# Block means of the values, made and sent in the pair's own first step

## The chip, the cores and the metric

The kernel runs on one core of one Trainium2 chip. The metric is the device time of one execution in microseconds, the median of several runs. The engines are named as the profile names them: PE (TensorE), DVE (VectorE), ACT (ScalarE), POOL (GpSimd) and SP (SyncE). Each works through its own list of instructions in order. An instruction that must wait for another engine holds everything behind it in its list.

## The reference

Three layers follow each other: an attention over 2 x 8 heads of 768 positions and 64 columns, a mixture of experts over the 1536 tokens (8 experts, two per token), and a dense layer with a leaky ReLU. The change touches only the attention:

```python
block, window = (32, 16)
k_sum = k.reshape(B, H, nb, block, D).max(axis=3)
v_sum = v.reshape(B, H, nb, block, D).mean(axis=3)
mask_l = np.abs(pos[:, None] - pos[None, :]) < window
scores_s = scale * np.einsum('bhsd,bhnd->bhsn', q, k_sum) + np.log(block)
...
a = softmax(np.concatenate([scores_l_m, scores_s], axis=-1))
return np.matmul(a, np.concatenate([v, v_sum], axis=2))
```

Each position attends to its near neighbours and to 24 block summaries. The summary of the values is their mean over 32 rows. These means are what the change is about.

## The kernel before

Two heads are a pair. There are 8 pairs (n = 0 to 7), and each has three steps (groups of four units of 64 positions), so 24 steps c = 3n, 3n+1, 3n+2. One step passes through five stages that are spread over neighbouring steps in the lists of the engines:

- `score(c)` on PE, line 1229: products of queries and keys.
- `softmax_max(c)` on DVE, lines 876 and 880: scale, mask and row maximum.
- `softmax_exp(c)` on ACT, line 666: four exponentials.
- `turn_probs(c)` on PE, line 1238, and `probs_out(c)` on ACT, line 674: transpose and copy out.
- `weigh(c)` on PE, line 1259: products with the values, then `normalise(c)` on DVE, lines 911 to 925.

Beside this, each pair has its queries and keys turned (`turn_q`, line 1186, `turn_k`, line 1195), the turned keys copied by ACT (`k_part`, lines 679 and 680) and the block maxima of the keys copied by ACT (`k_means`, line 685). From pair 2 on, `gate_turn` (line 1283) turns the results of an older pair for the router. It writes into the bank from which `k_part` reads, so it waits until the key copy of the next pair is done (`k_ready`).

The values of a pair lie in `v_win`, one of three buffers, with 120 rows: 64 own ones, 32 of the neighbours, and 24 block means. The means of pair n >= 1 travel like this. PE multiplies the values by a matrix of 1/32 (`block_means`, line 1207, 8 instructions at the head of a `score`). DVE copies the sums out (line 885, behind the row maximum). ACT issues three small transfers of 8 rows each (`means_out`, line 696), which bring them to the right rows. POOL spreads them over the units of `v_win` (line 582, in `finish_windows`). `weigh(3n)` waits for that (`windows_ready`). The table `MEANS_AT` says in which step the means of each pair are made.

Three queues matter around it. POOL's list is: for each pair, two copies of neighbour rows (lines 577, 579), the spread, then pieces of the first expert's weights, which are split into two parts (lines 528, 530). Two pieces stand behind the spreads of pairs 5 and 7, one behind those of pairs 2, 3, 4 and 6. SP loads the values of pair n+2 when `weigh(3n-1)` is done, then queries, keys and weights. At the end of the attention SP waits until the means of pair 7 have landed, and loads the noise and six more pieces of weights behind that.

Of the kernel before, what the change touches and what calls it, by code (L numbers as in the profile page):

```python
# [29 lines left out]
PAIRS = B * H // 2  # L30
# [3 lines left out]
GROUPS = UNITS // GU  # L34
# [6 lines left out]
BANK = 512  # L41
MEANS_COL = 256
MEAN_LOADS = 3
MEANS_AT = {2: 1} | {GROUPS * n - 2: n for n in range(2, PAIRS)}
THIRD = UNITS // 4
MASKED = -1e9
EPS = 1e-9
# [27 lines left out]
def build(nc, q, k, v, w_gate, w_noise, noise, w1, w2, w_in, w_out, out):  # L75
    ctx = ExitStack()
    with ctx:
# [580 lines left out]
        def _(act):  # L658
# [3 lines left out]
            def softmax_exp(c):  # L662
                b = c % 2
                act.wait_ge(max_ready, c + 1)
                for u in range(GU):
                    last = nc.scalar.activation(probs[:, b, u, :], scores[:, b, u, :], ACT.Exp, bias=negmax[:, b, u:u + 1])  # L666
                last.then_inc(probs_ready, 1)

            def probs_out(c):
                b = c % 2  # L670
                act.wait_ge(probs_turned, c + 1)
                if c >= 2:
                    act.wait_ge(weighed, c - 1)
                nc.scalar.copy(probsT[:, b, :], t_bank[b][0:KC, :]).then_inc(probsT_ready, 1)

            def k_part(n):

                act.wait_ge(k_turned, n + 1)
                nc.scalar.copy(kT[:, n % 2, :, 0:AFTER], k_own_after)
                nc.scalar.copy(kT[:, n % 2, :, AFTER:WK], k_ahead).then_inc(k_ready, 1)  # L680

            def k_means(n):

                act.wait_ge(k_max_done, n + 1)
                nc.scalar.copy(kT[:, n % 2, :, WK:KC], k_max[:].unsqueeze(1).to_broadcast([P, UNITS, NB])).then_inc(k_max_ready, 1)

            def means_out(n):

                act.wait_ge(means_copied, n)
                if n > VBUF:  # L690
                    act.wait_ge(windows_ready, n - VBUF)
                row, put = mean_parts[:].ap[0][0], mean_rows[:].ap[0][0]
                for u in range(THIRD):
                    of = bass.AP(mean_parts, (n % 2 * THIRD + u) * 2 * D, [[16 * row, 8], [1, 2 * D]])
                    to = bass.AP(mean_rows, (WK + 8 * u) * put + n % VBUF * 2 * D, [[put, 8], [1, 2 * D]])
                    act.dma_start(to, of).then_inc(means_loaded[n % VBUF], 16)

            def gate_xT(m, first=0, end=TPB):

                cols = slice(first * P, end * P)  # L700
                nc.scalar.copy(xT_gate[:, cols], turned[:, cols]).then_inc(gate_xT_ready, 1)
# [6 lines left out]
            for n in range(PAIRS):  # L708
                c = GROUPS * n
                if c >= 1:  # L710
                    probs_out(c - 1)
                softmax_exp(c)
                if c - 1 in MEANS_AT:
                    means_out(MEANS_AT[c - 1])
                if n == 0:
                    act.wait_ge(first_means_done, 1)
                    nc.scalar.copy(v_win[WK:KC, 0, :, :, 0:D], first_mean_bank.rearrange("x (h d) -> x h d", h=2).unsqueeze(2).to_broadcast([NB, 2, UNITS, D])).then_inc(first_means_ready, 1)
                elif n + 1 < PAIRS:
                    k_part(n + 1)

                probs_out(c)
                softmax_exp(c + 1)
                if c + 1 - 1 in MEANS_AT:
                    means_out(MEANS_AT[c + 1 - 1])
                if n == 0:
                    k_part(1)
                if n >= 2:
                    act.wait_ge(gate_turned, n - 1)
                    act.wait_ge(gate_multiplied, n - 2)
                    gate_xT(n - 2)  # L730

                probs_out(c + 1)
                if n + 1 < PAIRS:
                    k_means(n + 1)
                softmax_exp(c + 2)
                if c + 2 - 1 in MEANS_AT:
                    means_out(MEANS_AT[c + 2 - 1])
            act.wait_ge(gate_turned, PAIRS - 1)
            act.wait_ge(gate_multiplied, PAIRS - 2)
            gate_xT(PAIRS - 2)  # L740
# [858 lines left out]
```

## Time and profile before

| What | Value |
|---|---|
| Median of 3 runs | 788.01 us (785.98 to 790.22) |
| Profiled execution, its own time | 780.19 us |
| Span in the trace | 778.6 us |
| PE busy | 757.3 us, 97% of the span |
| DVE, ACT, POOL busy | 262.1, 230.2 and 368.8 us |
| Attention stage, from the trace | about the first 103 us |

The page of the profile gives averages over three stages that have little in common. The attention fills the first eighth of the span. In it the work of a step passes from PE to DVE to ACT and back. In the rest of the span PE works almost without a gap. An instruction in the rows below is read as start, length, engine, line, operation, what it writes and reads, and how many were merged. The brackets say how long its engine stood idle before it, and what ended that. `ACTq` rows are transfers that ACT's sequencer issues, and their length is the time that the issue takes, not the transfer.

### The profile page before, as it was taken

What the parts mean: (1) busy time and instruction counts of PE and PEld (TensorE: products, weight loads), DVE (VectorE), ACT (ScalarE), POOL (GpSimd) and SP (SyncE); (2) the same over time, 40 slices, a digit from 0 to 9 for tenths busy, and PEclk for the clock granted to TensorE, in tenths of its full rate; (3) what the DMA queues carried; (4) which work ended last, traced back from release to release, by engine and by line L of the source; (5) the groups of instructions that cost most, each with busy time, mean ns of one, the idle gap of its engine ahead of it and who ended that gap; (6) DMA issues with size and microseconds to landing.
All of it is one profiled execution on the core that took longest, in us unless ns stands there. A gap on an engine that the chain in (4) does not pass through costs nothing.

```text
span 778.6 us, 13087 instructions
## 1 busy us (share of the span) xinstructions
PE 757.3 (97%) x4497; PEld 619.8 (80%) x4498; DVE 262.1 (34%) x457; ACT 230.2 (30%) x384; POOL 368.8 (47%) x313
## 2 busy tenths in 40 slices
PE   8888899999999999999999999999999999999998
PEld 6666667788888888888888888888888888888886
DVE  2787772122221212222122221165443334332223
ACT  3677772212212122221212212144222222221221
POOL 5277836579787687879388852810110001000000
PEclk8899999999999999999999999999999999999999
DMA  9699766983544526262544612261110101010001
GB/s 183 124 243 218 219 225 211 338 289 121 183 154 99 212 93 207 90 215 95 175 162 139 200 65 61 88 231 53 29 54 28 54 4 51 0 54 0 0 1 54
DMA packets 77041, 97.74 MB, mean 126 GB/s; under 512 B 45768, under 2 KB 49008, under 8 KB 76976
## 3 DMA queue, kind: packets, MB, share of 16 engines
q1 hardware_dynamic: 58832, 45.52, 21.0%
q0 software_dynamic: 12464, 43.79, 17.6%
q10 hardware_dynamic: 5712, 7.99, 2.8%
q8 instruction: 21, 0.34, 0.2%
q14 instruction: 12, 0.10, 0.0%
HBM read 75.43 MB, written 23.59 MB: 127 GB/s over the span
## 4 chain that ended last, share of the span: by engine, by line
PE 90%; DVE 3%; DMA 2%; ACT 2%; SPq 1%; issue 1%; ACTq 0%; DVEq 0%
PE p L1426 43%; PE p L1531 6%; PE p L1533 6%; PE p L1532 6%; PE p L1546 5%; PE p L1548 5%; PE p L1547 5%; PE p L1418 3%; DMA v_win<-in_v 2%; PE p L1413 2%; PE p L1381 1%; ACT scores L666 1%; DVE scores L876 1%; PE p L1238 1%; PE p L1229 1%
## 5 line engine op out<-in xcount | busy, mean ns | idle before, releaser
L565 POOL TENSOR_TENSOR w_lo<-stage,w_hi 128x1024 fp32r<-128x1024 f32 x56 | 134.1, 2395 | 4.7
L1426 PE MATMUL p<-w_hi,hT_hi 128*128 x240 | 96.5, 402 | 0.0
L1426 PE MATMUL p<-w_hi,xT_hi 128*128 x240 | 96.1, 400 | 0.3 <-DVE xT_lo L1071 0.3
L1426 PE MATMUL p<-w_lo,hT_hi 128*128 x240 | 93.9, 391 | 0.0
L652 POOL DMA_INDIRECT y_pick<-y_by_tile,slots x20 | 19.2, 959 | 157.6 <-PE p L1518 132.4
L1426 PE MATMUL p<-w_lo,xT_hi 128*128 x240 | 93.6, 390 | 0.0
L1426 PE MATMUL p<-w_hi,hT_lo 128*128 x240 | 93.6, 390 | 0.0
L1426 PE MATMUL p<-w_hi,xT_lo 128*128 x240 | 93.5, 390 | 0.0
L1531 PE MATMUL p<-f_xT_hi,w_hi 128*128 (+2 forms) x200 | 77.2, 386 | 0.8 <-DVE f_xT_lo L1115 0.8
L796 ACT CAST hT_hi<-p 128x1024 fp32r<-128x1024 f32 x30 | 30.5, 1016 | 155.7 <-PE p L1418 155.7
L1533 PE MATMUL p<-f_xT_hi,w_lo 128*128 (+2 forms) x200 | 76.2, 381 | 0.0
L1532 PE MATMUL p<-f_xT_lo,w_hi 128*128 (+2 forms) x200 | 76.2, 381 | 0.0
L1546 PE MATMUL p<-w_hi,f_hT_hi 128*128 128x512 f32 x192 | 74.8, 390 | 0.1
L1548 PE MATMUL p<-w_hi,f_hT_lo 128*128 128x512 f32 x192 | 74.7, 389 | 0.0
L1547 PE MATMUL p<-w_lo,f_hT_hi 128*128 128x512 f32 x192 | 74.7, 389 | 0.0
L1123 DVE SCALAR_TENSOR_TENSOR f_h<-p,f_h 128x512 f32<-128x512 f32 x48 | 33.2, 691 | 119.9 <-ACT f_h L826 119.9
L1071 DVE TENSOR_TENSOR xT_lo<-p,xT_hi 128x512 fp32r<-128x512 f32 x31 | 21.4, 691 | 147.5 <-ACT xT_hi L793 147.5
L791 ACT ACTIVATE h_row<-p 128x1024 f32<-128x1024 f32 x30 | 30.8, 1027 | 135.6 <-PE p L1426 129.5
L826 ACT COPY f_h<-p 128x512 f32<-128x512 f32 x48 | 28.2, 588 | 143.3 <-PE p L1533 143.3
L563 POOL TENSOR_SCALAR w_hi<-stage 128x1024 fp32r<-128x1024 f32 x56 | 59.2, 1057 | 15.1 <-DMA stage<-in_moe_w 12.4
L1077 DVE COPY y_row<-p 128x512 f32<-128x512 f32 x31 | 21.5, 694 | 116.7 <-PE p L1426 116.7
L1426 PEld LDWEIGHTS p<-w_lo,hT_hi 128*128 128x128 f32 x240 | 45.0, 188 | 10.0
(231 smaller groups left out, 1288.1 us busy)
## 6 DMA issues: line engine op xcount, KB each, us to landing
stage<-in_moe_w POOLq DMA_DIRECT2D x48, 512.0 KB, 4.2
w_land<-in_moe_w SPq DMA_DIRECT2D x16, 512.0 KB, 5.6
y_by_tile<-y_row ACTq DMA_DIRECT2D x29, 256.0 KB, 2.0
x_by_tile<-x_ring SPq DMA_DIRECT2D x28, 256.0 KB, 4.9
x_row<-x_by_tile SPq DMA_DIRECT2D x28, 256.0 KB, 3.2
v_win<-in_v SPq DMA_DIRECT2D x8, 384.0 KB, 5.7
x_tokens<-x_out SPq DMA_DIRECT2D x12, 256.0 KB, 5.6
out<-f_y SPq DMA_DIRECT2D x9, 256.0 KB, 2.0
```

Of the source, the lines that this page charges most:

```text
L563: pool.tensor_scalar(w_hi[:, par, cols], stage[:, c % STAGES, :], 1.0, 1.0, ALU.mult, ALU.mult).then_inc(hi_split, 1)
L565: pool.tensor_tensor(w_lo[:, par, cols], stage[:, c % STAGES, :], w_hi[:, par, cols].bitcast(F32), ALU.subtract).then_inc(lo_split, 1)
L791: nc.scalar.activation(h_row[:], h_bank[:], ACT.Relu).then_inc(h_ready, 1)
L796: nc.scalar.copy(hT_hi[:].rearrange("p c m -> p (c m)"), hT_bank[:]).then_inc(hT_hi_ready, 1)
L1123: nc.vector.scalar_tensor_tensor(out=h, in0=f_h_bank[c % 2], scalar=0.01, in1=h, op0=ALU.mult, op1=ALU.max).then_inc(f_leaky_done, 1)
L1426: last = nc.tensor.matmul(bank, a, w, start=(c == 0 and i == 0), stop=(c == left_hi.shape[1] - 1 and i == 2))
L1531: nc.tensor.matmul(to, hi, f_xT_hi[:, cols], start=(k == 0), stop=False)
L1532: nc.tensor.matmul(to, hi, f_xT_lo[:, cols], start=False, stop=False)
L1533: last = nc.tensor.matmul(to, lo, f_xT_hi[:, cols], start=False, stop=(k == KD - 1))
L1546: nc.tensor.matmul(f_y_bank[m], f_hT_hi[:, c % 2, rows], hi, start=(c == 0), stop=False)
L1547: nc.tensor.matmul(f_y_bank[m], f_hT_hi[:, c % 2, rows], lo, start=False, stop=False)
L1548: last = nc.tensor.matmul(f_y_bank[m], f_hT_lo[:, c % 2, rows], hi, start=False, stop=(c == FC - 1))
```

## The change

The table of steps is new, and ACT now looks up the current step instead of the one before. Nothing else is changed.

```diff
-MEANS_AT = {2: 1} | {GROUPS * n - 2: n for n in range(2, PAIRS)}
+MEANS_AT = {GROUPS * n: n for n in range(1, PAIRS)}
...
                 softmax_exp(c)
-                if c - 1 in MEANS_AT:
-                    means_out(MEANS_AT[c - 1])
+                if c in MEANS_AT:
+                    means_out(MEANS_AT[c])
...
                 probs_out(c)
                 softmax_exp(c + 1)
-                if c + 1 - 1 in MEANS_AT:
-                    means_out(MEANS_AT[c + 1 - 1])
...
                 softmax_exp(c + 2)
-                if c + 2 - 1 in MEANS_AT:
-                    means_out(MEANS_AT[c + 2 - 1])
```

Before, the means of pair 1 were made in step 2 and those of pair n >= 2 in step 3n-2, and their transfers were issued one step later, behind the exponentials of step 3 and of step 3n-1. Now both happen in step 3n. The lists of POOL and SP are the same as before.

PE's list before, around the means of pair 5 (line 1207) in step 13; line 1229 is a score and line 1259 a weighing, line 1283 the gate turn:

```order
L1207 MATMUL p<-v_win,half_sums 32x192 x8
L1229 MATMUL p<-kT,qT 64x120 x8
L1238 MATMUL p<-ident,scores 120x128 x4
L1283 MATMUL p<-ident,x_out 128x128 x6
L1259 MATMUL p<-v_win,probsT 64x65 x8
L1229 MATMUL p<-kT,qT 64x120 x8
L1238 MATMUL p<-ident,scores 120x128 x4
L1186 MATMUL p<-ident,qk_nat 128x128 x6
L1259 MATMUL p<-v_win,probsT 64x65 x8
L1229 MATMUL p<-kT,qT 64x120 x8
```

PE's list in the changed kernel, the same place (its lines are numbered 4 lower, so 1203 are the means, 1225 a score, 1279 the gate turn):

```order
L1225 MATMUL p<-kT,qT 64x120 x8
L1234 MATMUL p<-ident,scores 120x128 x4
L1279 MATMUL p<-ident,x_out 128x128 x6
L1255 MATMUL p<-v_win,probsT 64x65 x8
L1225 MATMUL p<-kT,qT 64x120 x8
L1234 MATMUL p<-ident,scores 120x128 x4
L1182 MATMUL p<-ident,qk_nat 128x128 x6
L1255 MATMUL p<-v_win,probsT 64x65 x8
L1203 MATMUL p<-v_win,half_sums 32x192 x8
L1225 MATMUL p<-kT,qT 64x120 x8
```

The eight products of the means of pair 5 stood before `score(13)` and now stand before `score(15)`, the first of their own pair.

ACT's list before, from the third step of pair 4 into pair 5 (line 666 are the exponentials, 696 the three issues, 679 and 680 the key copy, 674 the probabilities):

```order
L685 COPY kT<-k_max 128x12x24
L666 ACTIVATE scores<-scores,negmax 128x120 x4
L696 DMA mean_rows<-mean_parts 8x128 x3
L674 COPY probsT<-p 120x512
L666 ACTIVATE scores<-scores,negmax 128x120 x4
L679 COPY kT<-p 128x12x80
L680 COPY kT<-p 128x12x16
L674 COPY probsT<-p 120x512
L666 ACTIVATE scores<-scores,negmax 128x120 x4
L701 COPY xT_gate<-p 128x768
```

ACT's list in the changed kernel, the same place:

```order
L685 COPY kT<-k_max 128x12x24
L666 ACTIVATE scores<-scores,negmax 128x120 x4
L674 COPY probsT<-p 120x512
L666 ACTIVATE scores<-scores,negmax 128x120 x4
L696 DMA mean_rows<-mean_parts 8x128 x3
L679 COPY kT<-p 128x12x80
L680 COPY kT<-p 128x12x16
L674 COPY probsT<-p 120x512
L666 ACTIVATE scores<-scores,negmax 128x120 x4
L701 COPY xT_gate<-p 128x768
```

The three issues stood between the exponentials of step 14 and the copy-out of that step's probabilities. Now they stand between the exponentials of step 15 and the key copy of pair 6.

## Rows read from the trace of the kernel before

**Rows 1.** Timeline of PE, pair 5: start us, busy us, instruction, count.

```profile
66.39 0.64 PE L1229 MATMUL p<-kT,qT 64*64 64x120 f32 x16
...
69.93 0.86 PE L1207 MATMUL p<-v_win,half_sums 64*32 64x192 f32 x16
70.72 0.64 PE L1229 MATMUL p<-kT,qT 64*64 64x120 f32 x16
71.29 0.65 PE L1238 MATMUL p<-ident,scores 128*120 128x128 f32 x4
71.78 0.82 PE L1283 MATMUL p<-ident,x_out 128*128 128x128 f32 x6
72.53 0.69 PE L1259 MATMUL p<-v_win,probsT 120*64 120x65 f32 x16
...
74.89 0.85 PE L1186 MATMUL p<-ident,qk_other 128*128 128x128 f32 x6
75.67 0.69 PE L1259 MATMUL p<-v_win,probsT 120*64 120x65 f32 x16
76.28 0.64 PE L1229 MATMUL p<-kT,qT 64*64 64x120 f32 x16
```

**Rows 2.** Timeline of PE: the two means that waited for values.

```profile
60.05 0.86 PE L1207 MATMUL p<-v_win,half_sums 64*32 64x192 f32 x16 [1.69 <-DMA v_win<-in_v]
...
80.50 0.86 PE L1207 MATMUL p<-v_win,half_sums 64*32 64x192 f32 x16 [0.61 <-DMA v_win<-in_v]
```

**Rows 3.** Timeline of PE: means of pair 2, first score of pair 2.

```profile
27.60 1.50 PE L1207 MATMUL p<-v_win,half_sums 64*32 64x192 f32 x16
...
34.83 0.64 PE L1229 MATMUL p<-kT,qT 64*64 64x120 f32 x16
```

**Rows 4.** Timeline of DVE: the copy of pair 5's means.

```profile
62.81 0.55 DVE L885 COPY mean_parts<-p 128x384 f32<-128x384 f32 x1
```

**Rows 5.** Timeline of ACT: issues of pair 1, key copies 2 and 3.

```profile
27.37 1.18 ACTq L696 DMA_DIRECT2D mean_rows<-mean_parts  x2
28.60 0.96 ACT L679 COPY kT<-p 128x960 f32<-128x960 f32 x1 [1.19 <-issue]
...
39.02 0.94 ACT L679 COPY kT<-p 128x960 f32<-128x960 f32 x1
```

**Rows 6.** Timeline of PE: a gate turn that awaits the key copy.

```profile
40.32 0.85 PE L1283 MATMUL p<-ident,x_out 128*128 128x128 f32 x6 [0.21 <-ACT kT L680]
```

**Rows 7.** Timeline of ACT: last issue of pairs 4, 5 and 7.

```profile
55.93 0.57 ACTq L696 DMA_DIRECT2D mean_rows<-mean_parts  x1
...
67.57 0.57 ACTq L696 DMA_DIRECT2D mean_rows<-mean_parts  x1
...
88.03 0.57 ACTq L696 DMA_DIRECT2D mean_rows<-mean_parts  x1
```

**Rows 8.** Timeline of POOL: the spread for pairs 1, 4, 5, 6, 7.

```profile
29.79 1.48 POOL L582 TENSOR_SCALAR v_win<-mean_rows 24x1536 f32<-24x1536 f32 x1 [14.62 <-DMA mean_rows<-mean_parts]
...
60.83 1.48 POOL L582 TENSOR_SCALAR v_win<-mean_rows 24x1536 f32<-24x1536 f32 x1 [2.53 <-DMA mean_rows<-mean_parts]
...
70.27 1.47 POOL L582 TENSOR_SCALAR v_win<-mean_rows 24x1536 f32<-24x1536 f32 x1 [1.38 <-DMA mean_rows<-mean_parts]
...
82.16 1.48 POOL L582 TENSOR_SCALAR v_win<-mean_rows 24x1536 f32<-24x1536 f32 x1
...
91.37 1.48 POOL L582 TENSOR_SCALAR v_win<-mean_rows 24x1536 f32<-24x1536 f32 x1 [1.16 <-DMA mean_rows<-mean_parts]
```

**Rows 9.** Timeline of PE, the ends of pairs 6 and 7.

```profile
85.27 0.69 PE L1259 MATMUL p<-v_win,probsT 120*64 120x65 f32 x16
...
86.55 0.64 PE L1229 MATMUL p<-kT,qT 64*64 64x120 f32 x16
...
94.08 0.69 PE L1259 MATMUL p<-v_win,probsT 120*64 120x65 f32 x16
```

**Rows 10.** Busy us of PE, PEld, DVE, ACT, POOL; PEclk, DMA share, GB/s.

```profile
55.00:60.00 5.00, 2.78 (x58) 2.15 (x50) 3.32 (x10) 3.81 (x11) 3.14 (x3) 1.00 1.24 225
```

## The prediction

> **What bounds the kernel now.** I read the page first, then the chain of waits, then the timelines of PE, DVE, ACT and POOL over the first 103 us. After that stretch PE is busy almost without a gap, so whatever the attention gains or loses is passed on in full to the end. In the attention no engine is full. A pair goes round a ring: PE makes scores, DVE masks them and takes maxima, ACT takes exponentials, PE turns and weighs. An undisturbed pair takes 9.89 us from its first score at 66.39 to that of the next one at 76.28 [rows 1].
>
> Two are longer, because the values for the means of pairs 5 and 7 had not landed. PE idled 1.69 and 0.61 us there [rows 2]. These 2.30 us lie on the chain of waits. The transfers of the means do not, they land before `weigh(3n)` needs them.
>
> I count in pairs. S(n) is the time at which PE starts the first score of pair n, or, in the changed kernel, the means in front of it.
>
> **The change part by part.** Instructions are neither added nor removed. What moves is eight products, one copy, three issues.
>
> *Waits for values.* These values landed at 60.0 and 80.4, and the means that need them now start beyond 64 and 87. This takes the 2.30 us away.
>
> *First pairs.* Pair 1's means leave the score of step 2 (0.79 us start to start, 69.93 to 70.72 [rows 1]). Pair 2's leave step 4, where they cost 1.4 of the 1.50 us that they take at the low clock [rows 3]. One set comes in at step 3, 0.79. ACT's key copy for pair 2 already stands behind three issues there [rows 5], and now waits a little longer for the copy of the sums. That makes 0.79 + 1.4 - 0.79 - 0.2 = 1.2 us gained. Bounds: 0 and 2.2. So S(2) moves from 34.83 [rows 3] to 33.6.
>
> *Products on PE, copy on DVE.* Now at the head of the first score. From the start of the products to the end of the copy is 62.81 + 0.55 - 60.05 = 3.31 us [rows 2, 4]. The products fill time in which PE would wait for exponentials anyway.
>
> *Issues on ACT.* The decisive part. Before, the three issues of pairs 2 to 7 stood behind the exponentials of a third step, and beside them PE was turning probabilities for which ACT had to wait anyway. Now the key copy stands behind them. The trace has this arrangement once, in step 3: two issues take 1.18 us, and the key copy starts 1.19 us late with nothing else to wait for [rows 5]. One issue is thus 0.57, one every 0.61. In the changed kernel they begin when the sums are copied: S + 3.31 + 0.06 = S + 3.37. The last begins at S + 4.59 and ends at S + 5.16, and the key copy starts at S + 5.2. The gate turn, which awaits the copy, starts 40.32 - 39.02 = 1.30 us later, at S + 6.5 [rows 5, 6]. From there PE has, start to start, gate turn 0.75, weigh 0.61, score 0.57, turn of probabilities 0.49, turn of queries 0.78, weigh 0.61 [rows 1], together 3.82. So a pair takes 10.32 us instead of 9.89: +0.43 for each of pairs 2 to 6. `weigh(3n)` is due at S + 9.71. In pair 6, without a turn of queries, it is due at S + 8.93. Bounds of the hold per pair: 0, if exponentials elsewhere cover it, and 1.2 [rows 5]. I take the replay.
>
> *Landing.* From the start of the last issue until POOL starts the spread, the trace has 4.90, 2.70 and 3.34 us for pairs 4, 5 and 7 [rows 7, 8], and about 1.8 for pair 1, whose issues fell into a quiet stretch [rows 5, 8]. The low end is 1.8, the high end 4.90, and I take 3.3 as the nearest to the middle two. Then the spread starts at S + 7.9, takes 1.48 [rows 8], and `weigh(3n)` can go at S + 9.45. For pairs 2 to 5 this hides behind S + 9.71 by 0.26.
>
> *POOL's list.* Pair 6 doesn't hide. Between the spreads of pairs 5 and 6 stand two weight pieces and two row copies, and from one to the other POOL took 82.16 - 70.27 = 11.89 us without waiting [rows 8]. Before, the spread of pair 6 still ended 1.6 us ahead of `weigh(18)` at 85.27 [rows 8, 9]. Now that of pair 5 starts 4 us later in its pair, so that of pair 6 starts at S(5) + 7.93 + 11.89 and `weigh(18)` goes at S(5) + 21.35. It would be due at S(5) + 10.32 + 8.93 = 19.25. A new wait of 2.1 us.
>
> *Pair 7.* Before, `weigh(21)` came 94.08 - 86.55 = 7.53 us after S(7) [rows 9]. Pair 7 has no key copy and no turns of keys and queries, so nothing covers the means. They are ready at S(7) + 9.45. 1.9 us more, and the spread becomes the last wait of the stage.
>
> *The sum.* S(5) = 33.63 + 3 x 10.32 = 64.6, before 66.39 [rows 1]. S(7) = 64.6 + 21.35 + 1.28 (from `weigh(18)` to the score, 86.55 - 85.27 [rows 9]) = 87.2, before 86.55. `weigh(21)` at 87.2 + 9.45 = 96.7, before 94.08. That is +2.6 us. Read another way: -1.2 first pairs, -2.3 waits for values, +2.1 key copies (five pairs), +2.1 POOL in pair 6, +1.9 pair 7. SP's loads behind the means of pair 7 start later by the same and a little more. So do ACT's casts of them, and I take nothing for it.
>
> The profiled execution took 780.19, so the sum gives 782.8 for such a one. The median of the runs is 7.8 above it. I add the shift as it stands: 788.0 + 2.6 = 790.6. A measurement here tells about 0.5% (3.9 us) from no change, so this shift lies inside.
>
> **The rivals.**
>
> *Transfers land late.* At 4.90 us, `weigh(3n)` goes at S + 11.0, 1.3 beyond its due time, in pairs 2, 3 and 4 (3.9), and pairs 6 and 7 lose 1.6 each: 2.6 + 7.1 = +9.7 in full, some +6.5 if it is so in most pairs, 794.5. For it: the queries, keys and weights that SP issues in the same stretch. Against: only one of four landings was like this.
>
> *The clock falls.* The products of pair 2 took 1.50 us at the low level, 1.2 GHz, against 0.86 at the high one, 2.4 GHz [rows 2, 3]. PE would now idle over 2 us before `weigh(18)`. If the clock falls once for some 7 us, as it did around that row, it costs up to 3 us: about 793. Against: from 55 to 60 PE was busy for only 2.78 of 5 us, with an idle time of 1.69 behind it, at a granted clock of 1.00 [rows 2, 10]. The Trainium skill's "TensorE: Matmul & The Clock Gate", Part 1, says that idleness throttles the array to 1.2 GHz and activity releases it. That fits the row of pair 2 and would make this rival's time, not the forecast's.
>
> *Faster.* The means cost only what nobody waits for, and the waits for values were the price. This needs transfers that land in 1.8 us, which takes 1.5 off each of pairs 6 and 7 (2.6 - 3.1 = -0.5), first pairs at their best bound (another -1.0), and key copies covered elsewhere (-1.7 over pairs 2 to 5): -3.2, 784.8. It decides if POOL's spread of pair 5 starts within 6 us of S(5). Only the quiet landing speaks for it.
>
> *No difference.* Gains and new waits cancel. At 2.0 us of landing the sum is 2.6 - 2 x 1.3 = 0.0: 788.0. The Trainium skill's "DMA: Bandwidth & Descriptors", section on the anatomy of one DMA, gives a fixed cost of about 2.0 us to a transfer, whatever its size; by it these 4 KB transfers would land like this. The rows of pairs 4, 5 and 7, at 2.70 and more, speak against it.
>
> **How the numbers follow.** Forecast (key copies and spreads late, +1.3 with landings of 2.7 to +4 with mixed ones): 0.48. Late landings: 0.20. Clock: 0.12. Faster: 0.10. No difference: 0.10. Slower by over 0.5%: 0.08 of the forecast's tail, 0.17 of the late landings, 0.08 of the clock, 0.33 together. Faster by over 0.5%: half of the faster rival and a little of chance, 0.06. Within: 0.61. The range must leave out no more than 2 in 10: from 786.5, between the faster rival and no difference, to 796, near the full price of late landings. The forecast's own range is 789.3 to 792.
>
> **What would show it.** Right: no wait of `block_means` for values; the key copy of pairs 3 to 7 starting behind the last issue, some 1.0 us later in its pair than before, with PE idle before the gate turn; POOL's spread of pair 6 starting 11.9 us after that of pair 5 without idle time, and PE waiting for it before `weigh(18)` and again before `weigh(21)`. Wrong: key copies that start right behind the exponentials, landings over 4 us, a granted clock below 1 after 33 us, or a stage that ends before 103 us.

## The result and the profile after

The changed kernel takes 796.5 us (795.1 to 798.8, 4 runs) beside 787.0 us for the kernel before (785.5 to 790.2). The ratio is 1.0116, 95% interval 1.0093 to 1.0139: it is 9.1 us slower, between 7.3 and 10.9. A second set of runs gave 1.0127 (1.0099 to 1.0155). The forecast was 790.6, or +2.6 us.

The page of the changed kernel, its span, PE's busy time and the granted clock in 40 slices:

```profile
span 797.2 us, 13082 instructions
...
PE 760.1 (95%) x4497; PEld 623.2 (78%) x4498; DVE 265.5 (33%) x457; ACT 229.2 (29%) x384; POOL 368.8 (46%) x313
...
PEclk9988999799999999999999999999999999999999
```

The clock line has a 7 and several 9s in its first slices; one slice is 20 us and hides what happens in 5. The stretches show it. Here are those of the changed kernel (columns as in [rows 10], the third last number is the granted clock):

```profile
30.00:35.00 5.00, 5.00 (x63) 3.78 (x61) 3.17 (x7) 2.15 (x7) 2.21 (x2) 0.67 1.19 292
40.00:45.00 5.00, 5.00 (x64) 4.01 (x62) 3.02 (x7) 3.03 (x10) 4.75 (x4) 0.66 0.42 73
55.00:60.00 5.00, 2.95 (x44) 1.98 (x48) 1.79 (x5) 1.31 (x5) 4.31 (x3) 0.72 1.19 208
60.00:65.00 5.00, 5.00 (x71) 3.98 (x64) 2.19 (x6) 2.51 (x6) 3.38 (x3) 0.59 0.62 165
75.00:80.00 5.00, 2.57 (x25) 2.04 (x22) 2.35 (x4) 3.58 (x8) 0.32 (x1) 0.77 0.71 236
```

From 25 us on the kernel before had a low clock once, from 25 to 33 us (0.58 and 0.74 in its two stretches), and 1.00 in every stretch from 35 us on. Now it falls four times to 1.2 GHz, for 3 to 7 us each, the first time in place of that earlier fall. (A low clock at 10 to 20 us comes and goes from profile to profile: 0.71 and 0.61 in the kernel before, 1.00 in this profile, 0.74 and 0.58 in its repeat h1.) What PE did before each fall, and when it was through with pairs 2 and 5 (the means at 45.00 and 82.97), is in its timeline:

```profile
29.47 0.71 PE L1234 MATMUL p<-ident,scores 128*120 128x128 f32 x4 [2.60 <-ACT scores L666]
...
39.69 1.07 PE L1279 MATMUL p<-ident,x_out 128*128 128x128 f32 x6 [1.99 <-ACT kT L680]
...
45.00 0.86 PE L1203 MATMUL p<-v_win,half_sums 64*32 64x192 f32 x16
...
51.50 0.84 PE L1279 MATMUL p<-ident,x_out 128*128 128x128 f32 x6 [1.59 <-issue]
...
57.05 1.00 PE L1255 MATMUL p<-v_win,probsT 120*64 120x65 f32 x16 [2.28 <-POOL v_win L582]
57.98 1.50 PE L1203 MATMUL p<-v_win,half_sums 64*32 64x192 f32 x16
...
77.65 1.47 PE L1279 MATMUL p<-ident,x_out 128*128 128x128 f32 x6 [2.43 <-issue]
...
82.97 0.86 PE L1203 MATMUL p<-v_win,half_sums 64*32 64x192 f32 x16
...
93.11 0.69 PE L1255 MATMUL p<-v_win,probsT 120*64 120x65 f32 x16 [1.04 <-POOL v_win L582]
...
102.14 0.69 PE L1255 MATMUL p<-v_win,probsT 120*64 120x65 f32 x16 [0.21 <-POOL v_win L582]
```

Idle times of 2.60, 1.99, 2.28 and 2.43 us stand ahead of the four falls. The rows of 51.50 and 93.11 have 1.59 and 1.04 us, and the clock stayed up behind them. The length of the idle time alone doesn't tell: in h1, a repeat below, the clock was low behind an idle time of 1.67 us, and in e1 it stayed up behind one of 2.07 us. The waits for values [rows 2] are gone. The gate turn (line 1279) waits for the key copy as in [rows 6], but for 1.6 to 2.4 us in place of 0.21 (not in pair 4, where PE itself was late at the low clock). `weigh` (line 1255) waits for POOL's spread in pairs 3 and 6, and for 0.21 us in pair 7. Means at the low clock take 1.50 us (57.98), as pair 2's did [rows 3]. `weigh(21)`, at 94.08 before [rows 9], comes at 102.14.

ACT in pair 3 shows the hold, as in [rows 5]: two more issues, then the key copy, 1.09 us late with nothing else to wait for.

```profile
48.97 1.20 ACTq L696 DMA_DIRECT2D mean_rows<-mean_parts  x2
50.22 0.96 ACT L679 COPY kT<-p 128x960 f32<-128x960 f32 x1 [1.09 <-issue]
```

POOL's spreads answer to [rows 8]. The brackets tell which one waited for the transfers. I call the time from the start of the last issue to the start of the spread the landing; where POOL comes late by itself, it is only an upper bound:

```profile
39.19 1.48 POOL L582 TENSOR_SCALAR v_win<-mean_rows 24x1536 f32<-24x1536 f32 x1 [6.90 <-DMA mean_rows<-mean_parts]
...
55.52 1.47 POOL L582 TENSOR_SCALAR v_win<-mean_rows 24x1536 f32<-24x1536 f32 x1 [8.29 <-DMA mean_rows<-mean_parts]
...
79.68 1.47 POOL L582 TENSOR_SCALAR v_win<-mean_rows 24x1536 f32<-24x1536 f32 x1 [6.23 <-DMA mean_rows<-mean_parts]
...
91.59 1.47 POOL L582 TENSOR_SCALAR v_win<-mean_rows 24x1536 f32<-24x1536 f32 x1
...
100.61 1.47 POOL L582 TENSOR_SCALAR v_win<-mean_rows 24x1536 f32<-24x1536 f32 x1 [0.97 <-DMA mean_rows<-mean_parts]
```

The last issues of pairs 2 to 7 began at 37.4, 49.6, 63.6, 75.8, 87.6 and 98.8 (the row of pair 4, at 65.39, is left out). So the landings took 1.8, 5.9, 1.8, 3.9, at most 4.0, and 1.8 us. From 79.68 to 91.59 are 11.91 us without a gap: POOL's list holds pair 6, as forecast.

One more loss stands behind the attention. DVE's first routing operation took 0.29 us before and 1.85 us after (0.26 us in e3, where it overlaps nothing on POOL). First the two rows of the kernel before, DVE and POOL:

```profile
103.59 0.29 DVE L980 SCALAR_TENSOR_TENSOR r_sc<-logits 128x96 f32<-128x96 f32 x1
```

```profile
101.40 2.36 POOL L541 TENSOR_TENSOR w_lo<-w_land,w_hi 128x1024 fp32r<-128x1024 f32 x1
```

And of the changed kernel:

```profile
111.25 1.85 DVE L976 SCALAR_TENSOR_TENSOR r_sc<-logits 128x96 f32<-128x96 f32 x1
```

```profile
110.64 2.35 POOL L541 TENSOR_TENSOR w_lo<-w_land,w_hi 128x1024 fp32r<-128x1024 f32 x1
```

POOL's subtraction ends at 112.99 and DVE's operation at 113.10. From the last logits on PE (103.51 before, 111.17 after) to the first gather (118.37 and 127.58) the changed kernel takes 1.55 us more. A gather is POOL's first transfer of token rows for the experts.

### The profile page after: what moved, and what is told of

The parts are those of the page before. It is cut to its first block, busy times and chain, and to the rows that moved or that the text cites. A ratio compares the mean times of both kernels' runs of the same rounds, so it can differ in the third digit from the quotient of the medians.

```text
span 797.2 us, 13082 instructions
## 1 busy us (share of the span) xinstructions
PE 760.1 (95%) x4497; PEld 623.2 (78%) x4498; DVE 265.5 (33%) x457; ACT 229.2 (29%) x384; POOL 368.8 (46%) x313
## 4 chain that ended last, share of the span: by engine, by line
PE 88%; DVE 3%; issue 2%; POOL 2%; DMA 2%; ACT 2%; ACTq 1%; SPq 0%; POOLq 0%; DVEq 0%
PE p L1422 42%; PE p L1527 6%; PE p L1529 5%; PE p L1528 5%; PE p L1542 5%; PE p L1544 5%; PE p L1543 5%; PE p L1414 4%; PE p L1409 2%; DMA mean_rows<-mean_parts 1%; PE p L1255 1%; ACT scores L666 1%; POOL v_win L582 1%; PE p L1203 1%; PE p L1225 1%
## 5 line engine op out<-in xcount | busy, mean ns | idle before, releaser
L1422 PE MATMUL p<-w_hi,hT_hi 128*128 x240 | 96.6, 402 | 0.0
L1422 PE MATMUL p<-w_hi,xT_hi 128*128 x240 | 96.6, 402 | 0.0
L1422 PE MATMUL p<-w_hi,hT_lo 128*128 x240 | 93.5, 390 | 0.0
L1119 DVE SCALAR_TENSOR_TENSOR f_h<-p,f_h 128x512 f32<-128x512 f32 x48 | 33.2, 691 | 120.1 <-ACT f_h L822 120.1
L563 POOL TENSOR_SCALAR w_hi<-stage 128x1024 fp32r<-128x1024 f32 x56 | 59.1, 1056 | 13.8 <-DMA stage<-in_moe_w 11.1
L518 POOL DMA_DIRECT2D stage<-in_moe_w x48 | 31.7, 666 | 49.0 <-PE p L1422 28.8
```

The costliest lines, as they stand in the source:

```text
L518: pool.dma_start(stage_view(c % STAGES, c), source(c)).then_inc(staged[c % STAGES], 16)
L563: pool.tensor_scalar(w_hi[:, par, cols], stage[:, c % STAGES, :], 1.0, 1.0, ALU.mult, ALU.mult).then_inc(hi_split, 1)
L1119: nc.vector.scalar_tensor_tensor(out=h, in0=f_h_bank[c % 2], scalar=0.01, in1=h, op0=ALU.mult, op1=ALU.max).then_inc(f_leaky_done, 1)
L1422: last = nc.tensor.matmul(bank, a, w, start=(c == 0 and i == 0), stop=(c == left_hi.shape[1] - 1 and i == 2))
```

## The experiments

All start from the changed kernel unless said otherwise. The table has S(2) to S(7), the start of the means at the head of the pair's first score (for the kernel before, e2, e3 and g1 of that score itself), and `weigh(21)`, in us, from one profile each, and the ratio of times to the kernel before from the same job.

| Kernel | pair 2 | 3 | 4 | 5 | 6 | 7 | weigh(21) | ratio (95%) |
|---|---|---|---|---|---|---|---|---|
| before | 34.8 | 44.5 | 54.8 | 66.4 | 76.3 | 86.6 | 94.1 | 1 |
| b_again, before again | 36.0 | 45.2 | 55.6 | 66.5 | 76.4 | 86.0 | 93.5 | 0.9998 (0.9981-1.0016) |
| forecast | 33.6 | 44.0 | 54.3 | 64.6 | 74.9 | 87.2 | 96.7 | 1.0033 |
| changed | 32.5 | 45.0 | 58.0 | 70.3 | 83.0 | 94.3 | 102.1 | 1.0116 (1.0093-1.0139) |
| h1, changed again | 34.1 | 45.8 | 57.9 | 68.1 | 79.7 | 92.8 | 102.3 | 1.0127 (1.0099-1.0155) |
| e1 key copy first | 32.6 | 42.9 | 54.7 | 64.3 | 75.7 | 88.5 | 98.2 | 1.0102 (1.0064-1.0141) |
| e2 old steps | 35.2 | 46.6 | 58.6 | 68.2 | 78.5 | 90.9 | 99.0 | 1.0096 (1.0070-1.0122) |
| e3 step 3n-1 | 33.1 | 43.2 | 53.3 | 63.3 | 73.4 | 83.5 | 90.4 | 0.9984 (0.9967-1.0002) |
| g1, e3 again | 33.3 | 43.4 | 53.5 | 63.6 | 73.6 | 83.7 | 90.6 | 0.9985 (0.9973-0.9997) |
| e4 fillers | 31.4 | 42.0 | 55.4 | 68.1 | 79.9 | 92.3 | 101.2 | 1.0070 (1.0044-1.0096) |
| f2 loads later | 33.2 | 45.3 | 55.6 | 66.2 | 76.5 | 88.8 | 97.0 | 1.0083 (1.0060-1.0105) |
| f3 POOL's order | 32.3 | 41.9 | 55.2 | 67.0 | 77.0 | 86.7 | 97.3 | 1.0104 (1.0081-1.0127) |
| f4 more fillers | 33.4 | 44.1 | 57.2 | 67.4 | 78.8 | 91.0 | 98.9 | 1.0104 (1.0076-1.0132) |
| g2 one-input split | 31.4 | 43.5 | 56.7 | 68.9 | 81.1 | 91.7 | 99.5 | 1.0084 (1.0070-1.0098) |
| g3 e1 and f2 | 32.4 | 41.9 | 51.9 | 64.9 | 76.8 | 87.7 | 97.4 | 1.0068 (1.0048-1.0088) |
| h2 f2 and fillers | 33.4 | 44.1 | 54.5 | 65.6 | 76.6 | 88.3 | 96.6 | 1.0036 (1.0020-1.0052) |

Up to `weigh(21)` g2 is the changed kernel too, so that one kernel shows 102.1, 102.3 and 99.5 us there. A difference of less than 3 us between two single profiles shows little; the rows behind it have to carry it.

**e1, the key copy ahead of the issues.**

```diff
                 softmax_exp(c)
-                if c in MEANS_AT:
-                    means_out(MEANS_AT[c])
...
                 elif n + 1 < PAIRS:
                     k_part(n + 1)
+                if c in MEANS_AT:
+                    means_out(MEANS_AT[c])
```

> The changed kernel, but in step 3n ACT copies the keys of the next pair first and issues the three transfers of the means behind that. Theory H (the issues hold the key copy, PE idles before the gate turn, and the clock falls in that idle time): the key copy starts right behind the exponentials, the idle time of 1.6 to 2.4 us before the gate turn is gone, the low-clock stretches behind it too; the stage up to weigh(21), 8.1 us late in the changed kernel, is back by 3 to 5 us, and the time by 3 to 6 us, near 791. Rival L (late landing and POOL's list are all of the loss): the issues end about 1.1 us later still, so every spread is later, and the time grows by 1 to 4 us, to 798 to 800.

PE of e1, means of pairs 2 to 4, and two of the weighings that waited:

```profile
32.59 0.86 PE L1203 MATMUL p<-v_win,half_sums 64*32 64x192 f32 x16
...
42.91 0.86 PE L1203 MATMUL p<-v_win,half_sums 64*32 64x192 f32 x16
...
54.05 0.69 PE L1255 MATMUL p<-v_win,probsT 120*64 120x65 f32 x16 [2.07 <-POOL v_win L582]
54.67 0.86 PE L1203 MATMUL p<-v_win,half_sums 64*32 64x192 f32 x16
...
75.06 0.69 PE L1255 MATMUL p<-v_win,probsT 120*64 120x65 f32 x16 [1.70 <-POOL v_win L582]
```

No gate turn waits for more than 0.50 us any more and the clock stays at 1.00 from 20 to 75 us. `weigh(21)` is 4.0 us earlier than in the changed kernel. So the rows show that the issues hold the key copy, and with it PE. But the spread still comes late (2.07 and 1.70 us in the rows), since landings took 5.1 and 4.7 us in pairs 3 and 5, and the clock falls again at 77 and 87 us. The time, 1.0102 (1.0064 to 1.0141), can't be told from the changed kernel's; it is 793.3 us where some 791 was expected. The rival's fear, issues that end 1.1 us later, did not come true: the last issue of pair 2 began 4.9 us behind the means, as in the changed kernel. In the trace the second issue of pair 2 begins at 36.87 while the key copy runs from 36.62 to 37.56: ACT's sequencer issues transfers while a copy that was handed on before runs.

**e2, the old steps with the new place of the issues.**

```diff
-MEANS_AT = {GROUPS * n: n for n in range(1, PAIRS)}
+MEANS_AT = {2: 1} | {GROUPS * n - 2: n for n in range(2, PAIRS)}
...
-                if c in MEANS_AT:
-                    means_out(MEANS_AT[c])
+                if n >= 1:
+                    means_out(n)
```

> The kernel before in its steps (means made in 2 and 3n-2), only the issues stand where the changed kernel has them, behind the exponentials of step 3n and ahead of the key copy. The sums were copied long before, so the issues start with the exponentials. Theory H (the place of the issues): the key copy starts 0.6 to 0.8 us late, and there may be low-clock stretches; 2 to 5 us slower than the kernel before. Rival M (the step in which the products and the copy are made): as the kernel before within 1 us.

The place of the issues alone makes the kernel slower by 0.96% (0.70 to 1.22), 7.6 us, more than the 2 to 5 expected. `weigh(21)` is 4.9 us late. Weighings waited 0.90, 2.63 and 2.02 us for spreads in pairs 2, 3 and 6. In pairs 2 and 3 the transfers had landed after 4.9 and 6.3 us. In pair 6 it was POOL's list: its spread came 11.89 us behind that of pair 5, without a gap. In the kernel before the issues stood some 3 us earlier in a pair, and this distance covered landings up to 4.9 us. So most of the loss hangs on where the transfers are issued, not where the means are made. In this profile the clock was at 1.00 from 35 to 90 us: late spreads and late key copies cost 4.9 us here with hardly any help of the clock.

**e3 and g1, made and issued in step 3n-1.**

```diff
-MEANS_AT = {GROUPS * n: n for n in range(1, PAIRS)}
+MEANS_AT = {GROUPS * n - 1: n for n in range(1, PAIRS)}
...
                 softmax_exp(c + 2)
+                if c + 2 in MEANS_AT:
+                    means_out(MEANS_AT[c + 2])
```

> Means made in step 3n-1 and issued in the same step behind its exponentials, where ACT waits for PE anyway. The waits for values of 2.3 us should be gone (values landed at 60.0 and 80.4; these means start near 62.5 and 81), and neither the key copy nor the spread is late. Theory H: 1 to 3 us faster than the kernel before, about 785. Rival M (means near their own pair cost by themselves): not faster than before, or slower by the 0.8 us per pair that the products take there.

> e3 once more, to settle whether it beats the kernel before. In e3's profile the first gather was 3.1 to 3.4 us earlier than in the two profiles of the kernel before, but the times differed by 1.1 us only, with an interval that just touches no change. If the stage carries over, this run is again 1 to 3.5 us faster; if e3's profile was a lucky one, the difference is 0 to 1 us.

The means of pairs 6 and 7 of e3 on PE, without a wait in brackets:

```profile
69.94 0.86 PE L1203 MATMUL p<-v_win,half_sums 64*32 64x192 f32 x16
...
80.01 0.86 PE L1203 MATMUL p<-v_win,half_sums 64*32 64x192 f32 x16
```

The waits for values [rows 2] are gone, and none of PE's waits in pairs 3 to 6 is over 0.5 us. Pairs 2 to 6 take 10.1 us each. `weigh(21)` comes 3.7 us earlier than in the kernel before, and the first gather 3.1 to 3.4. The time gains only 1.2 us: 0.9984 (0.9967 to 1.0002), then 0.9985 (0.9973 to 0.9997). The second interval lies just below 1, so this version beats the kernel before, narrowly, and the changed one clearly. About 2 us of the earlier stage are lost again before the tiles run evenly, and where was not settled (see the end).

**e4 and f4, fillers.** Transposes of the identity into a free bank: 10 before the gate turns of pairs 2 to 6 in e4 (below) and 14 in f4, 14 before the turn of probabilities of step 4, and more before `weigh` of pairs 3 and 6 (f4 also 5).

```diff
+            def fill(count, i_bank):
+                for i in range(count):
+                    nc.tensor.transpose(t_bank[i_bank % 2][:, 0:P], ident[:], ident[:])
...
+                    if n < PAIRS - 1:
+                        fill(10, c + 1)
                     gate_turn(n - 2)
```

> The changed kernel with idle transposes of the identity matrix put into PE's gaps: 10 before the gate turn of pairs 2 to 6, 14 before the turn of probabilities of step 4, 8 before the weighing that awaits the spread in pairs 3 and 6. The waits themselves stay. Theory C (much of the loss is the clock): the granted clock stays at 1 from 25 to 100 us, the stage ends 3 to 5 us earlier than in the changed kernel, about 792 in time. Rival W (the waits alone are the loss and the low clock hides beside them): within 1 us of the changed kernel or slower by the fillers.

> As e4, with more idle transposes: 14 before each gate turn, 24, 10 and 18 before the weighings of pairs 3, 5 and 6. e4 still had the low clock at 55 to 63 and at 90 to 97 us. Theory C: the granted clock stays at 1 throughout, and the stage is 3 to 4 us shorter than in e4: the price of the clock is what is left between this kernel and the changed one, some 4 to 5 us. Rival W: the clock stays up and the stage is not shorter by more than 1 us, since the waits hide it.

From 25 us to the end of the attention e4 had the low clock only twice, f4 not at all. All of f4 from 25 to 100 us, then its gate turn of pair 2 and the means behind it:

```profile
25.00:100.00 75.00, 71.88 (x1172) 58.83 (x1170) 54.88 (x126) 49.86 (x128) 48.83 (x32) 1.00 0.74 177
```

```profile
40.26 0.84 PE L1279 MATMUL p<-ident,x_out 128*128 128x128 f32 x6 [0.45 <-ACT kT L680]
...
44.08 0.86 PE L1203 MATMUL p<-v_win,half_sums 64*32 64x192 f32 x16
```

From the gate turn to the next means are 3.82 us here, and 5.31 us in the changed kernel at the low clock (39.69 to 45.00; again 5.32 in pair 5, 77.65 to 82.97). So one such fall costs 1.5 us. Pair 2 as a whole takes 10.6 us instead of 12.5: 1.5, and 0.4 for the end of the fall before it. f4's `weigh(21)` is 3.3 us earlier than that of the changed kernel, less than the 4 to 5 expected. Pair 3 still takes 13.1 us: its transfers landed after 5.3 us, and 24 fillers held `weigh(9)` until 0.9 us behind the end of the spread, so the fillers cost time themselves. In time, f4 (1.0104) can't be told from the changed kernel and e4 (1.0070) is better. The fillers did hold the clock in the timed executions too: the median of their mean granted clocks is 0.990 in f4 and 0.992 in e4, 0.991 in the kernel before beside them and 0.983 in the changed kernel. The clock alone is thus worth some 0.5% of the time by e4 and nothing by f4. Why f4's 3.3 us in the profile don't show in its time at all stays open.

**b_again, the kernel before once more.**

> The kernel before once more, to see whether its first profile is typical. That execution took 780.2 us where its timed runs have 786.8, and in every other profile so far PE idles 8.4 us before the turn of tile 1's hidden row, while ACT starts its first h_row 18.7 us after the first gather, against 10.8 in that first profile. Theory S (that wait belongs to both kernels and the first profile alone is without it): the profile shows the 8.4 us wait and 785 to 789 us. Rival T (the kernel before does not have it, and the change brings it): no such wait, profile near 780.

787.1 us, ratio 0.9998 (0.9981 to 1.0016). Its profile has the long wait of ACT for tile 1's hidden row, which the first profile had not. More on this at the end.

**f2, loads behind the next pair's means.**

```diff
+                if 1 <= n < PAIRS - 2:
+                    sp.wait_ge(means_loaded[(n + 1) % VBUF], 16 * MEAN_LOADS * ((n + 3) // VBUF))
                 for e, c in PIECES_BESIDE[n]:
                     load_piece(e, c)
```

> The changed kernel, but SP issues the weight pieces and stores of iteration n (1 to 5) only when the means of pair n+1 have landed. Theory D (those 0.5 MB pieces and the stores ahead of the small transfers make them land late: 5.9 us in pair 3, 3.9 in pair 5, 1.8 elsewhere): all landings fall to about 1.8 us, the wait of weigh(9) for the spread (2.3 us) and its low clock go; the stage is 2 to 4 us shorter, unless POOL waits for its first piece. Rival R (the late landings come from queries, keys or the receipt): still over 3 us in pairs 3 and 5, no gain.

POOL's spreads of pairs 2 and 3 in f2. Their last issues began at 37.7 and 49.9:

```profile
39.52 1.47 POOL L584 TENSOR_SCALAR v_win<-mean_rows 24x1536 f32<-24x1536 f32 x1 [5.39 <-DMA mean_rows<-mean_parts]
...
51.69 1.47 POOL L584 TENSOR_SCALAR v_win<-mean_rows 24x1536 f32<-24x1536 f32 x1 [2.49 <-DMA mean_rows<-mean_parts]
```

PE of f2, the means of pairs 3 to 6 and `weigh(9)` between them:

```profile
45.31 0.86 PE L1205 MATMUL p<-v_win,half_sums 64*32 64x192 f32 x16
...
54.98 0.69 PE L1257 MATMUL p<-v_win,probsT 120*64 120x65 f32 x16
55.59 0.86 PE L1205 MATMUL p<-v_win,half_sums 64*32 64x192 f32 x16
...
66.21 0.86 PE L1205 MATMUL p<-v_win,half_sums 64*32 64x192 f32 x16
...
76.46 0.86 PE L1205 MATMUL p<-v_win,half_sums 64*32 64x192 f32 x16
```

Both landings took 1.8 us, that of pair 3 5.9 before the edit. `weigh(9)` doesn't wait, its low clock is gone, and pairs 3, 4 and 5 take 10.28, 10.62 and 10.25 us, where the prediction had 10.32. In pairs 4 and 5 the landings still took 3.0 and 2.8 us beside queries and keys, so not all fell to 1.8 as expected. `weigh(21)` is 5.1 us earlier than in the changed kernel. The time, 1.0083 (1.0060 to 1.0105), is lower too, but the intervals of the two still touch. Theory D holds for pair 3, for pieces and stores together; the run moved both and doesn't part them.

**f3, POOL's order, on e1.**

```diff
-            pieces_between = [(), (), (0,), (1,), (2,), (3, 4), (5,), (6, 7)]
+            pieces_between = [(), (), (0,), (1,), (2,), (3,), (4, 5), (6, 7)]
```

> As e1 (key copy ahead of the issues), and one weight piece is moved on POOL from behind the spread of pair 5 to behind that of pair 6. Theory P (POOL's list holds pair 6): the spread of pair 6 is no longer 11.9 us behind that of pair 5, the wait of 1.6 us before weigh(18) goes; that of pair 7 then comes 11.9 us after it, which leaves it at most 0.5 us late. Stage 1 to 2 us shorter than e1, time 791 to 792. Rival: the landing, not the list, holds pair 6: no change against e1.

Pair 6 takes 9.7 us instead of 12.8, so the list had held it. But the spread of pair 7 came 11.7 us behind that of pair 6, and `weigh(21)` waited 2.9 us for it. The wait moved, and there was no gain in time (1.0104), where 791 to 792 us was expected and 794.6 came. The expectation of at most 0.5 us late was wrong.

**g2, a split with one input.** The low part of weight piece 3 is left out.

```diff
+                if c == 3:
+                    pool.tensor_scalar(w_lo[:, 1, cols], w_land[:, 1, cols], 1.0, 1.0, ALU.mult, ALU.mult).then_inc(second_rest, 1)
+                else:
...
```

> The changed kernel, but POOL's last split before the gathers (the low part of weight piece 3 of expert 1) is a copy with one input and 1.05 us instead of the subtraction of 2.35 us; the low part is thus left out. In every profile so far the first routing operation of DVE (line 976, 0.26 us alone) ends 0.11 us after that subtraction of POOL when the two overlap: 1.85 us in the changed kernel. Theory K (the two operations exclude each other): that operation ends 1.3 to 1.6 us earlier relative to the last logits, the first gather as well, and the time is 1 to 1.5 us below the changed kernel's. Rival N (DVE waits for the noise or for ACT, and POOL's end is chance): it stays at 1.85 us.

DVE's operation in g2:

```profile
108.65 0.52 DVE L979 SCALAR_TENSOR_TENSOR r_sc<-logits 128x96 f32<-128x96 f32 x1
```

POOL's copy in g2:

```profile
108.02 1.04 POOL L542 TENSOR_SCALAR w_lo<-w_land 128x1024 fp32r<-128x1024 f32 x1
```

The copy ends at 109.06, the operation of DVE at 109.17. From the last logits to the first gather are 15.10 us, against 16.41 in the changed kernel and 14.86 in the one before. Theory K holds: DVE's operation, whose two inputs lie in SBUF, doesn't end until POOL's is done. In all fourteen profiles with an overlap it ended 0.11 to 0.12 us after POOL's, wherever it began. The Trainium skill ("SBUF — State Buffer", "SBUF: two separate sides") tells of a port pair that the two share as an exclusive lock, and these rows agree with it. The stage itself was 2.6 us shorter here than in the changed kernel (`weigh(21)` at 99.5), though the kernel is the same up to there, which is why the time (1.0084, 1.0070 to 1.0098) can't be laid to this edit.

**g3, e1 and f2 together.**

> The changed kernel with both edits: the key copy ahead of the issues (e1) and SP's pieces and stores behind the next pair's means (f2). e1 took 4.0 us from the stage up to weigh(21) and f2 5.1. Theory A (two separate causes beside each other): no idle time before the gate turns, no wait for the spread in pairs 2 to 5, a pair of some 10.0 us, no low clock in them; what stays is POOL's list in pair 6 and the uncovered spread of pair 7, so weigh(21) comes at 94 to 96 and the time is 788 to 791. Rival B (one cause in two guises): like the better of the two, 792 to 793.

Pairs 2 and 3 took 9.5 and 10.1 us, less than with either edit. Then SP's added wait held the queries of a later pair, PE waited 1.78 us for them and the clock fell. `weigh(21)` came at 97.4 and the ratio was 1.0068, 792.8 us. Theory A had 94 to 96 and 788 to 791; the time is that of rival B. The two causes are separate in the first pairs; the whole can't decide, since the edit brought a wait of its own.

**h1 and h2, the changed kernel again, and f2 with fillers.** h2 has f2's wait on SP and these fillers:

```diff
                 if n >= 2:
+                    if n < PAIRS - 1:
+                        fill(14, c + 1)
                     gate_turn(n - 2)
...
                 score(c + 2)
+                if n == 1:
+                    fill(14, c + 1)
...
+                if n == 6:
+                    fill(12, c)
                 weigh(c)
```

> The changed kernel once more. Its first profile had weigh(21) at 102.1 us, while g2, the same kernel up to there, had it at 99.5. If the stage varies from run to run with the landings and with the clock, this profile lies anywhere between, with the time 7 to 11 us above the kernel before.

> f2 (SP's pieces and stores behind the next pair's means) with idle transposes in PE's gaps: 14 before the gate turns of pairs 2 to 6, 14 before step 4's turn of probabilities, 12 before weigh(18). The issues still hold the key copy, POOL's list and the uncovered spread of pair 7 stay. Theory C (what the sum of the prediction left out is the low clock and late landings alone): clock 1 throughout, pairs 2 to 5 of 10.3 to 10.6 us each, weigh(21) at 95.5 to 97.5, which is the forecast's 96.7, and the time 3 to 5 us above the kernel before: 2.6 and the 1.5 of DVE behind POOL. Rival W (the clock costs nothing, since the waits hide it): weigh(21) as in f2, at 97.0 or later by the fillers, time 792.7 or more.

h1 repeats the changed kernel: `weigh(21)` at 102.3, ratio 1.0127, with three falls of the clock from 25 us on in place of four. h2 on PE, the means of pairs 2 to 7 and `weigh(21)`:

```profile
33.44 0.86 PE L1205 MATMUL p<-v_win,half_sums 64*32 64x192 f32 x16
...
44.07 0.86 PE L1205 MATMUL p<-v_win,half_sums 64*32 64x192 f32 x16
...
54.52 0.86 PE L1205 MATMUL p<-v_win,half_sums 64*32 64x192 f32 x16
...
65.59 0.86 PE L1205 MATMUL p<-v_win,half_sums 64*32 64x192 f32 x16
...
76.58 0.86 PE L1205 MATMUL p<-v_win,half_sums 64*32 64x192 f32 x16
...
88.31 0.86 PE L1205 MATMUL p<-v_win,half_sums 64*32 64x192 f32 x16
...
96.60 0.69 PE L1257 MATMUL p<-v_win,probsT 120*64 120x65 f32 x16 [0.43 <-POOL v_win L584]
```

And all of it from 25 to 100 us:

```profile
25.00:100.00 75.00, 70.06 (x1173) 56.49 (x1171) 55.71 (x130) 51.61 (x132) 51.03 (x33) 1.00 0.76 188
```

The clock is 1.00. `weigh(21)` comes at 96.60 and the forecast had 96.7. The time is 1.0036 (1.0020 to 1.0052), +2.8 us, and the forecast had +2.6. How close both come is partly luck. In h2 pairs 4 and 5 take 11.1 and 11.0 us in place of 10.3, pairs 6 and 7 11.7 and 8.3 in place of 12.3 and 9.5, and DVE's loss behind POOL (its operation took 1.88 us) is in the time and was not in the forecast. What the run does show is that with the low clock and the late landings of the large neighbours removed most of the distance is gone, nearly 6 us of `weigh(21)` and 7 us of time between h2 and h1 in the same job. Against f2 the fillers bring only 0.4 us at `weigh(21)` (97.0 to 96.6), so the 1.0083 of f2, from another job, and this 1.0036 don't give the price of the clock.

## Why the prediction was wrong

The direction was right, the size was not. 796.5 lies beyond the range's 796.

- *Waits for values:* right. No means wait for values in any profile with the new steps.
- *First pairs, -1.2:* right within a microsecond or so. S(2) was 32.5 and 34.1 in two profiles, forecast 33.6. The 32.5 had no low clock at 10 to 20 us, the 34.1 had one.
- *Issues hold the key copy, a pair of 10.32 us:* right where nothing disturbs it (10.28, 10.25 in f2), and e1 shows the cause. That PE would idle before the gate turns was right too.
- *POOL's list, 11.89 us between the spreads of pairs 5 and 6:* right, 11.91. But `weigh(18)` waited only 1.0 us for it in place of 2.1, since pair 5 was longer and gave POOL time: pair 6 took 11.3 us, forecast 12.3.
- *Pair 7, +1.9:* the mechanism was right, the size was not. From S(7) to `weigh(21)` are 7.9 us in place of 9.45, for the landing took 1.8 us; that is 0.4 more than before. In f2 and h2 it is 0.7 and 0.8 more.
- *Landing at 3.3 us in every pair:* the first step that failed. Measured were 1.8 in pairs 2, 4 and 7, but 5.9 in pair 3, outside my bound of 4.90, and 3.9 in pair 5. The bounds came from rows in which the issues stood elsewhere among SP's loads. In the new place pair 3's stood right behind two pieces of 512 KB and beside three stores. This one late landing costs 2.7 us (pair 3: 12.98 against 10.28 in f2).
- *The clock:* the second step that failed, and the larger one in this profile. The sum took nothing for it and the rival had 0.12, for one fall. The argument against, that 1.69 us of idle time left the clock at 1.00 [rows 2, 10], was drawn from one row, while the same sum put an idle time before every gate turn, whose length it didn't work out: 1.5 to 2.4 us were measured wherever PE wasn't late itself. It fell four times. The sum's 3.82 us behind the gate turn became 5.31 in pair 2 and 5.32 in pair 5, and pair 4, at the low clock from its start on, took 12.3 us, against 10.25 in f4. Late landings and the clock feed each other: either one removed takes 5.1 us (f2) or 3.3 us (f4) from `weigh(21)`, both together 5.5 (h2). How the time divides between the two is not shown: f4 has the clock at 1.00 and none of the gain in time, and e2 lost 7.6 us while its profile has no fall between 35 and 90 us.
- *The whole, at `weigh(21)`:* 102.1 against 96.7, 5.4 us more. Pairs 2 to 5 were 9.2 us longer than the sum had them: 1.9 by the clock in pair 2 and 0.3 by a key copy held somewhat longer, 2.7 by the landing in pair 3, 2.0 by the clock in pair 4, and 2.3 in pair 5, of which 1.5 by the clock and 0.8 because two of its issues took 2.03 us in place of 1.18. Against this S(2) was 1.2 us earlier, and pairs 6 and 7 were 1.0 and 1.6 shorter. So the error would have been larger without errors the other way.
- *What comes behind the attention:* the sum took nothing for it and missed 1.55 us (1.3 of it gone again in g2). It wasn't SP's loads or ACT's casts, which the prediction named: POOL's last split moved later against the stage and ran into DVE's first routing operation.

Against the kernel before, `weigh(21)` of the changed kernel is +8.1 us, and +9.2 at the first gather (127.58 against 118.37): DVE's 1.55 us, less 0.4 between `weigh(21)` and the last logits. The measured difference is +9.1. The two repeats agree: from b_again to h1 the first gather is 9.2 us later again (118.01 and 127.24).

## What to carry to other kernels

Work that an engine does while it would wait anyway is free there and may cost much one step further: three transfer issues of 0.6 us each cost nothing behind the exponentials of one step and held a whole ring behind those of the next. To remove a wait for an operand that lands late, move the consumer later by as little as lets the operand arrive; one step did what two overdid (e3 against the changed kernel). When a sum creates idle time on PE, work out how long it is in each place and price the low clock there, and take the landing time of a small transfer from what will be ahead of it in its new place, not from where it stood.

## What the runs showed of the hardware

A transfer of 4 KB within SBUF took 1.8 us from its issue to POOL's start in quiet stretches. With half-megabyte pieces issued just before it and stores beside it (pair 3) it took 5.1 to 6.5 us, in the eight profiles that have this arrangement. In the three with SP's pieces and stores behind it, the same transfer took 1.8 (f2), 2.1 (h2) and 3.4 us (g3).

ACT waits long for tile 1's hidden row in most profiles, in either kernel. The row of the changed kernel, of b_again and of h1, each from ACT's timeline:

```profile
147.72 1.02 ACT L787 ACTIVATE h_row<-p 128x1024 f32<-128x1024 f32 x1 [15.26 <-remote]
```

```profile
139.53 1.02 ACT L791 ACTIVATE h_row<-p 128x1024 f32<-128x1024 f32 x1 [16.62 <-remote]
```

```profile
138.16 1.02 ACT L787 ACTIVATE h_row<-p 128x1024 f32<-128x1024 f32 x1 [6.03 <-PE p L1441]
```

In h1, h2 and the first profile of the kernel before the wait is 6.0 us and what PE does next follows at once. In all others it is 12 to 18 us, and PE stands idle for 7 to 13 us in place of 0.7. In the job with h1 and h2, on another chip, the kernel before took 778.9 us, in the others 786.8 to 788.2. The releaser is given as "remote", so the profile doesn't say what it waits for. It belongs to neither kernel, and its size fits the 7 us by which the first profile lay under the median. It may be where e3's gain was lost: e3 and its repeat g1 are 0.3 us apart at the first gather and 4.5 us at this row, with waits of 13.8 and 18.0 us. That is not shown; no run here took the wait apart.
